# Fused attention and two expert layers on one core: zero rows and negated maxima in one transfer, x placed in two halves, early weights in every second step

## What is computed

```python
q_assign = argmax(q_n @ c_n.T); k_assign = argmax(k_n @ c_n.T)      # 16 clusters per head
scores = where(q_assign[:, None] == k_assign[None, :], q @ k.T / 8, -1e9)
attn = exp(scores - max(scores)); attn = attn / (sum(attn) + 1e-9)
x = heads_side_by_side(attn @ v)                                    # [1536, 512]
h = x @ w_in; P = a0 + a1*h + a2*h^2 + a3*h^3; Q = 1 + |b0||h| + |b1|h^2
y = (P / (Q + 1e-6)) @ w_out                                        # w_in [512, 2048]
out = ((y @ w1) * (y @ w2)) @ w3 @ w4                               # w1, w2 [512, 1024]
```

## Time and profile before

| | |
|---|---|
| median of three runs | 756.98 us (756.45 to 760.11) |
| the profiled execution | 757.19 us, of which the trace spans 755.4 us |
| TensorE matmul busy | 724.8 us, 96% of the span |
| TensorE weight load busy | 593.2 us, 79% |
| VectorE busy | 500.1 us, 66% |
| ScalarE busy | 423.1 us, 56% |
| GpSimd busy | 363.0 us, 48% |
| mean granted TensorE clock | 0.995 of full |

### The profile page before, as it was taken

One profiled execution on the slowest core, in us unless ns is written; L12 is line 12 of the kernel. 1 busy time (PEld: TensorE's weight loads), 2 busy tenths in 40 slices (PEclk: granted clock), 3 DMA queues, 4 the chain that ended last, 5 costly groups with the idle time before them and its releaser, 6 DMA issues.

```text
span 755.4 us, 12741 instructions
## 1 busy us (share of the span) xinstructions
PE 724.8 (96%) x4849; PEld 593.2 (79%) x4849; DVE 500.1 (66%) x796; ACT 423.1 (56%) x750; POOL 363.0 (48%) x271
## 2 busy tenths in 40 slices
PE   4899999999999999999999999999999999999998
PEld 2567667667677788888888888878779999998886
DVE  6888778778874577677767686775875555544211
ACT  4366666666665788878666686773433333223221
POOL 4068678768776646652222223441636466551000
PEclk9899999999999999999999999999999999999999
DMA  7334645444331442000000021103100100000111
GB/s 156 66 92 124 161 127 142 123 103 124 97 83 40 140 133 77 1 1 1 0 1 1 1 98 70 57 1 112 56 29 19 38 29 29 29 1 15 56 43 56
DMA packets 67132, 47.75 MB, mean 63 GB/s; under 512 B 30880, under 2 KB 59392, under 8 KB 67072
## 3 DMA queue, kind: packets, MB, share of 16 engines
q1 hardware_dynamic: 67072, 46.94, 22.5%
HBM read 28.35 MB, written 3.15 MB: 42 GB/s over the span
## 4 chain that ended last, share of the span: by engine, by line
PE 79%; SPq 12%; DVE 3%; DMA 2%; issue 2%; ACT 2%; POOL 0%; DVEq 0%; ACTq 0%
PE psum L1129 77%; SPq L1069 5%; SPq L1051 2%; SPq L1028 1%; DMA OPS<-NMT 1%; SPq L1042 1%; DMA OPS<-OPS 1%; SPq L1035 1%; DVE psum L1645 1%; SPq L1043 1%; PE psum L1134 1%; SPq L1053 1%; ACT P L1425 1%; DMA RAWQK<-in_k 1%; PE psum L663 1%
## 5 line engine op out<-in xcount | busy, mean ns | idle before, releaser
L1129 PE MATMUL psum<-OPS 128*128 128x384 f32 x576 | 129.9, 362 | 15.3 <-DMA OPS<-NMT 9.2
L1129 PEld LDWEIGHTS psum<-OPS 128*128 128x128 f32 x576 | 98.6, 194 | 48.1 <-issue 19.3
L541 POOL TENSOR_TENSOR G<-TT,G 128x512 fp32r<-128x512 f32 x48 | 62.3, 1299 | 151.6 <-ACT G L426 151.6
L1807 POOL TENSOR_TENSOR PSUMS<-PSUMS,P 128x768 f32<-128x768 f32 x64 | 108.2, 1690 | 17.1 <-ACT P L1425 8.7
L1425 ACT ACTIVATE P<-psum 128x768 f32<-128x768 f32 x96 | 76.4, 810 | 55.6 <-PE psum L1129 55.3
L1645 DVE TENSOR_REDUCE psum<-psum 128x1 f32<-128x768 f32 x90 | 86.5, 961 | 28.7 <-PE psum L1129 28.1
L1129 PE MATMUL psum<-G,WSPLIT 128*128 128x512 f32 x360 | 86.6, 390 | 1.1 <-POOL G L541 1.1
L1129 PE MATMUL psum<-XT,WSPLIT 128*128 128x512 f32 x360 | 86.5, 389 | 0.0
L471 DVE SCALAR_TENSOR_TENSOR HH<-UU,ABSB,psum 128x512 f32<-128x512 f32 x48 | 35.9, 748 | 69.0 <-ACT TT L404 68.9
L1129 PEld LDWEIGHTS psum<-G,WSPLIT 128*128 128x128 f32 x360 | 67.4, 188 | 15.5 <-POOL G L541 1.5
L1129 PEld LDWEIGHTS psum<-XT,WSPLIT 128*128 128x128 f32 x360 | 67.6, 188 | 14.0
(11 more groups left out here) (126 smaller groups left out, 1257.9 us busy)
## 6 DMA issues: line engine op xcount, KB each, us to landing
OPS<-OPS SPq DMA_DIRECT2D x32, 192.0 KB, 3.3
W3R<-in_moe_w SPq DMA_DIRECT2D x8, 512.0 KB, 3.8
RAWF<-in_moe_w SPq DMA_DIRECT2D x16, 256.0 KB, 3.3
RAWQK<-in_q SPq DMA_DIRECT2D x16, 192.0 KB, 3.2
RAWQK<-in_k SPq DMA_DIRECT2D x16, 192.0 KB, 3.9
V<-in_v SPq DMA_DIRECT2D x16, 192.0 KB, 2.9
XT<-XH SPq DMA_DIRECT2D x64, 48.0 KB, 2.0
XT<-XL SPq DMA_DIRECT2D x64, 48.0 KB, 2.0
```

The lines of the kernel that those rows point to most:

```text
L541: nc.gpsimd.tensor_tensor(G[:, n % 2, 1, :], TT[:, n % 4, :], G[:, n % 2, 0, :].bitcast(F32), ALU.subtract).then_inc(g_lo, 1)
L1129: return nc.tensor.matmul(o, stationary, moving, start=start, stop=stop, skip_group_check=True)
L1807: nc.gpsimd.tensor_tensor(total, P32[:, (2 * u) % 4, :, 0:QS] if n == 1 else total, P32[:, (2 * u + n) % 4, :, 0:QS], ALU.add).then_inc(p_ ...
```

## The change

`place_masks` loses its DMA of zeros. In its stead BQ is taken out of OPS into a tile of its own, BQS, in which the slots of units u and u + 2 (two slots of the same parity) lie side by side. NM becomes four groups of six columns; `negate_maxima(u)` writes one of the two halves of a pair, and the other half stays zero from a memset at the start. The transpose, the copy and the DMA of `place_maxima` carry both halves: twelve rows of 128 in place of six, so that one DMA writes the negated maxima of unit u and zeros for unit u + 2.

In SyncE's step `copy_rows` comes first, then the XH half of `place_x`, `load_v`, `place_maxima`, the XL half of `place_x`, `load_qk`, weights, masks. The early weights 1 to 5 are loaded in steps 1, 3, 5, 7, 9 (before: 1 to 5). As BQ has moved, the waits of the later weights change: tile 8 waits for the scores of unit 14, tile 9 for those of unit 15, and tile 9 is issued behind `place_x(14)`.

```diff
-            AQ, AK, BQ, BK = range(4)
+            AQ, AK, BK, BQ = range(4)
-            OPS = ph("OPS", [P, 4, 4, S], F32R)
+            OPS = ph("OPS", [P, 4, 3, S], F32R)
+            BQS = ph("BQS", [P, 2, 2, S], F32R)
-            NM = ph("NM", [P, 8], F32)
+            NM = ph("NM", [P, 2, 2, NT], F32)
...
+        def operand(slot, which):
+
+            return BQS[:, slot % 2, slot // 2, :] if which == BQ else OPS[:, slot, which, :]
...
-            return TP[0:NT, 0, 0:P] if 2 <= u <= UNITS - 2 else SM[0:NT, 0, 0:P]
+            return TP[0:2 * NT, 0, 0:P] if 2 <= u <= UNITS - 2 else SM[0:2 * NT, 0, 0:P]
...
+            if f == 8:
+                sp.wait_ge(st_ready, NT * (UNITS - 1))
             if f == 9:
-                sp.wait_ge(st_ready, NT * (UNITS - 1))
-            if f == 10:
                 sp.wait_ge(st_ready, NT * UNITS)
...
-                sp.dma_start(OPS[96:97, u % 4, BQ, :].bitcast(F32), OPS[97:98, u % 4, BQ, :].bitcast(F32)).then_inc(mask_rows, 16)
...
-                sp.dma_start(OPS[96:97, u % 4, BQ, :].rearrange("j (n w) -> j n w", n=NT).bitcast(F32),
-                             NMT[0:NT, :].bitcast(F32)).then_inc(nm_rows, 16)
-
-            def place_x(u):
+                sp.dma_start(BQS[96:97, u % 2].rearrange("j s (n w) -> j (s n) w", n=NT).bitcast(F32),
+                             NMT[0:2 * NT, :].bitcast(F32)).then_inc(nm_rows, 16)
+
+            def place_x(u, parts=((0, XH), (1, XL))):
...
             def step(u):
-                if has(u - 2):
-                    place_x(u - 2)
                 if has(u + 3):
                     copy_rows(u + 3)
+                if has(u - 2):
+                    place_x(u - 2, ((0, XH),))
                 load_v(u + 1)
                 place_maxima(u + 1)
+                if has(u - 2):
+                    place_x(u - 2, ((1, XL),))
                 if has(u + 5):
                     load_qk(u + 5)
-                if u < EARLY_W:
-                    load_weights(sp, u, ld_w[u])
+                if u % 2 == 1 and u < 2 * EARLY_W - 2:
+                    load_weights(sp, (u + 1) // 2, ld_w[(u + 1) // 2])
                 if has(u + 3):
                     place_masks(u + 3)
...
-            load_later_weights(sp, 9)
             place_x(UNITS - 2)
-            for f in range(10, 14):
+            for f in range(9, 14):
                 load_later_weights(sp, f)
...
-                        pe.wait_ge(mask_rows, 80 * (u - DIRECT + 1))
+                        pe.wait_ge(mask_rows, 64 * (u - DIRECT + 1))
...
-                nc.tensor.transpose(turn_bank(u), NM[:, 0:NT], IDENT).then_inc(nm_turned, 1)
+                nc.tensor.transpose(turn_bank(u), NM[:, u // 2 % 2].rearrange("p s n -> p (s n)"), IDENT).then_inc(nm_turned, 1)
...
-                nc.scalar.copy(NMT[0:NT, :], turn_bank(u)).then_inc(nm_copied, 1)
+                nc.scalar.copy(NMT[0:2 * NT, :], turn_bank(u)).then_inc(nm_copied, 1)
...
+            nc.vector.memset(NM, 0.0).then_inc(nm_cleared, 1)
...
-                nc.vector.tensor_scalar(NM[:, 0:NT], rows, -1.0, CAP, ALU.mult, ALU.min).then_inc(nm_ready, 1)
+                nc.vector.tensor_scalar(NM[:, u // 2 % 2, u // 2 % 2], rows, -1.0, CAP, ALU.mult, ALU.min).then_inc(nm_ready, 1)
...
-                nc.gpsimd.memset(OPS[96:P, slot, BQ:BK + 1, :].bitcast(F32), 0.0).then_inc(ops_const, 1)
+                nc.gpsimd.memset(operand(slot, BQ)[96:P].bitcast(F32), 0.0)
+                nc.gpsimd.memset(operand(slot, BK)[96:P].bitcast(F32), 0.0).then_inc(ops_const, 1)
```

More of the change, by code:

```diff
@@ L98, in build @@
             VMEAN = ph("VMEAN", [P, 2], F32)
-            NM = ph("NM", [P, 8], F32)
-            ph("GAP_P", [P, 39 + 207], F32)
+            NM = ph("NM", [P, 2, 2, NT], F32)
+            ph("GAP_P", [P, 39 + 207 - 16], F32)
             ph("GAP_HH", [P, 5 * CH], F32)
@@ L197, in build @@
         nm_ready = sem("nm_ready")
+        nm_cleared = sem("nm_cleared")
         nm_turned = sem("nm_turned")
@@ L1041, in copy_rows @@
                 slot = u % 4
-                sp.dma_start(OPS[0:D, slot, BQ, :].bitcast(F32), OPS[0:D, slot, AQ, :].bitcast(F32)).then_inc(b_rows[slot], 16)
+                sp.dma_start(operand(slot, BQ)[0:D].bitcast(F32), OPS[0:D, slot, AQ, :].bitcast(F32)).then_inc(b_rows[slot], 16)
                 sp.dma_start(OPS[0:D, slot, BK, :].bitcast(F32), OPS[D:P, slot, AK, :].bitcast(F32)).then_inc(b_rows[slot], 16)
@@ L1050, in place_masks @@
                         part = (2 * side + x) * QUAD
-                        sp.dma_start(OPS[D:D + QUAD, u % 4, which, x * HALF:(x + 1) * HALF].bitcast(F32),
+                        sp.dma_start(operand(u % 4, which)[D:D + QUAD, x * HALF:(x + 1) * HALF].bitcast(F32),
                                      MROWS[part:part + QUAD, :].bitcast(F32)).then_inc(mask_rows, 16)
-                sp.dma_start(OPS[96:97, u % 4, BQ, :].bitcast(F32), OPS[97:98, u % 4, BQ, :].bitcast(F32)).then_inc(mask_rows, 16)
             def place_maxima(u):
@@ L1059, in place_maxima @@
                     sp.wait_ge(ops_const, 2 * 4)
-                sp.dma_start(OPS[96:97, u % 4, BQ, :].rearrange("j (n w) -> j n w", n=NT).bitcast(F32),
-                             NMT[0:NT, :].bitcast(F32)).then_inc(nm_rows, 16)
-            def place_x(u):
+                sp.dma_start(BQS[96:97, u % 2].rearrange("j s (n w) -> j (s n) w", n=NT).bitcast(F32),
+                             NMT[0:2 * NT, :].bitcast(F32)).then_inc(nm_rows, 16)
+            def place_x(u, parts=((0, XH), (1, XL))):
                 sp.wait_ge(x_done, u + 1)
                 to = slice(u % 2 * D, u % 2 * D + D)
-                for e, src in ((0, XH), (1, XL)):
+                for e, src in parts:
                     for g in range(4):
@@ L1137, in ops @@
             def ops(u, which):
-                return OPS[:, u % 4, which, :]
+                return operand(u % 4, which)
             def sides(u):
@@ L1383, in ops2 @@
             def ops2(u, which, rows=slice(0, P)):
-                return OPS[rows, u % 4, which, :].rearrange("p (h n) -> p h n", h=2)
+                return operand(u % 4, which)[rows].rearrange("p (h n) -> p h n", h=2)
             def round_q(u):
@@ L1404, in scale_masks @@
                     if u > DIRECT:
-                        act.wait_ge(mask_rows, 80 * (u - DIRECT))
+                        act.wait_ge(mask_rows, 64 * (u - DIRECT))
                     last = nc.scalar.activation(MROWS, SIM, ACT.Copy, scale=BIG_ROOT)
@@ L1648, in negate_maxima @@
                 rows = MROW0 if u == 0 else MROW
+                if u == 0:
+                    dve.wait_ge(nm_cleared, 1)
                 dve.wait_ge(sm_free, NT * (u + 1))
```

## The result

The changed kernel takes 747.82 us (median, 747.38 to 748.13), the kernel before in the same runs 756.72. The ratio is 0.9877, interval 0.9849 to 0.9904. Forecast was 748.0. The profiled execution took 748.09 us (forecast for it: 748.3) with a span of 746.3. One of the six executions of the later run `e9_cen_later` took 4041.28 us, for which there is no trace; its ratio leaves it out.

The account below looks back on a forecast made before the run. SyncE's DMA queue, slower per attention step than TensorE's 13.5 us, was taken as the bound. 757.19 - 9.2 of waits + 0.3 gave 748.3 profiled, 748.0 against the median, range 746.8 to 751.8.

Parts of the forecast that it names:

- What bounds: Attention: SyncE's queue step, 14.82 us with weights and 13.59 without, exceeds TensorE's 13.5, so the maxima's DMA is late.
- Zero row, order and weights: SyncE's step: 0.64 us less per step, maxima 2.64 us earlier, weights spread to 27.13 us a pair against 26.96.
- Maxima before XL: SyncE's step: the maxima's DMA is issued 1.1 us early at worst, so all eight waits go, 9.2 us.
- The transfer of twelve rows: DMA of the negated maxima: taken as 2.40 us, between 2.1 and 2.9, with 0.83 us of issue.
- The masks: Needed by `score_max(u + 3, 0)` at 11.80 us, landing at 10.07, or 11.14 with the stall; 0.7 to 1.7 left.
- rival 3: Attention: masks become the bound and the kernel slower, 764.5 us if they land 1.5 us late; chance 0.04.
- Rival 2: TensorE's wait for the maxima is the transfer's own 2.40 us, so all eight waits stay, 756.5 to 757; chance 0.06.
- the rule of the cheap dispatch: SyncE's queue: issuing is cheap, some 50 ns, so taking 13 issues away gives under 1 us and the maxima stay late.
- Costs taken as nothing: Transpose 0 to 1.3 us, copy at most 0.26 again, memsets and later weights: each taken as 0.

Follow-up runs that it names:

- e9_cen_later: The changed kernel with q and k of unit 0 loaded ahead of the centroids; 748.1 us, ratio 0.9866.
- e7: The changed kernel with one more DMA of 3 KB behind the maxima in steps 1 to 12; 751.03 us, ratio 0.9918.
- e8: The changed kernel with two more DMAs of 3 KB a step behind the maxima in steps 1 to 12; 756.66 us, ratio 0.9996.
- e3: The kernel before with only the zero row merged into the transfer of the maxima, old order and weights' steps; 753.2 us, ratio 0.9948.
- e4: The changed kernel with the early weights back in steps 1 to 5; 749.17 us, ratio 0.989.
- e5: The changed kernel with SyncE's step in the old order, both halves of x ahead of the maxima; 753.84 us, ratio 0.9953.
- e6: The changed kernel with both halves of x behind the maxima; 762.14 us, ratio 1.0056.
- e2: The kernel before with only the early weights moved to steps 1, 3, 5, 7, 9; 757.88 us, ratio 1.0002.
- e10: The changed kernel as it is, run again; 747.41 us, ratio 0.9859.
- e1: The kernel before with only the new order of SyncE's step; 751.33 us, ratio 0.9912.

## Why the prediction was right, point by point

*What bounds: the queue's step against TensorE's 13.5.* Right for the steps with weights, where the queue had no pause of over 0.2 us from 78 to 134 us and four waits made 5.3 of the 9.2 us. Misread for the steps without: the prediction took 13.59 against 13.5 as a lateness that stays, but ahead of the three waits there, and of that at 74.46, the queue had stood idle for MROWS, and these 3.8 us come from the place of the maxima behind the masks and x. The change removes both, since it shortens the list by 0.64 us and this path by 0.64 + 2.64; that both came out of one forecast is in part luck. Adding 0.6 us a step costs 3.2 us in all, 1.2 us a step brings back the old time (e7, e8, by way of the masks); taking 0.64 away alone gives 3.9 us (e3, 757.12 to 753.2).

*Zero row, order and weights.* The sum was right, and the parts were not priced one by one. By their effect alone they are 3.9 (zero row), 5.8 (order: 757.12 to 751.33) and nothing that can be told; the first two together 7.9 (e4) and not 9.7, as they act on the same eight waits.

*Maxima before XL, 1.1 us of margin in the heaviest case.* The queue's part was right: the DMA was issued 96.23 - 82.46 = 13.77 us after the last copy's end, forecast 14.18 at worst, and in all steps from 55 us on it left within 0.63 us of its own copy's end. That x must be split is shown by e5 (waits for the maxima) and e6 (waits at `score_max(u + 2, 0)`).

*The transfer of twelve rows, taken at 2.40, bounded by 2.9.* Mis-sized in its upper end. Where TensorE was stopped by it, the time from issue to restart can be read. In the traces of e3, e5, e7 and the changed kernel there are fifteen such cases: nine lie from 2.30 to 2.54, six at 3.05, 3.33, and 3.86 to 4.10. With six rows, in sixteen cases of the kernel before and of e2, it was 2.04 to 2.43. In e10 there is one more, of 3.59. (Only transfers that stopped TensorE can be read so, and those of the changed kernel stop it only when they take over 4 us, so these counts don't tell how often a landing is late.) At 4.10 the margin is gone, which is the one wait of 0.2 in the changed kernel: issued at 123.06, TensorE went on at

```profile
127.16 0.62 PE L1135 MATMUL psum<-BQS,OPS 128*128 128x384 f32 x2 [0.21 <-DMA BQS<-NMT]
```

The forecast came out since the DMA is issued early enough in all steps; it stood nearer to the edge than the text said. Four of the late ones (3.86, 3.90, 3.94, 4.10) are the same transfer, issued between 123 and 126.1 us, in four kernels, which speaks for something else that runs there; twice the rows as the cause was not tested either. So this stays open. The issue itself cost 0.82 for 0.78, as taken.

*The masks, landing at 10.07 to 11.14 against 11.80.* The mechanism was right, the landing too short: I took the median of 2.1. In the changed kernel the last one is issued at 90.4, 7.9 after the copy (forecast 7.97), and the masks of that step take 2.7 to 3.2 to land, so that the last is there between 10.6 and 11.1, with 0.7 to 1.2 of margin and not 1.7. Steps without weights have up to 3.1, so the 512 KB of weights ahead are not shown to be the reason. In the step of 163.31 the margin was gone: with stalls in XL and k the last mask was issued 9.2 after the copy's end, and TensorE started `score_max` at 175.35, 12.04 after it and not 11.80. That is the wait of 0.3. The bound of 11.14 was therefore too low, and the change runs at this edge as well. e6, 2.6 us later, is over it: rival 3 is a real mechanism. That my price for it (1.5 us in each of eleven steps, 764.5) was near what e6 showed (762.14) is luck, for e6 has five waits of 0.2 to 3.3 us and a slower clock behind some of them.

*Rival 2 and the rule of the cheap dispatch.* Rival 2 is refuted by the result and by e1: the waits for NMT went while the transfer got no shorter. The rule is refuted by e7 and e8: a DMA holds this queue for about 0.6 us whatever its size (0.58 for 3 KB, 0.60 for 192 KB), and that of twelve rows onto one partition for 0.82. By the Trainium skill's "usually small relative to the DMA itself" ("DMA: Bandwidth & Descriptors", section "Issuing engines are not separate DMA queues") the added DMAs would change little; the traces disagree, with 0.58 us of issue beside median landings of 2.0 (e7) and 1.7 (e8) for these DMAs, and the time rose by 3.2 and 8.8 us. The 50 ns that the prediction takes from that page of the Trainium skill stand there for DMAs issued from GpSimd, and these are issued from SyncE.

*Costs taken as nothing.* The transpose with twelve columns took 85 ns of weight load for 83, the copy 257 for 255, and the later weights brought no wait after attention.

## What to carry to other kernels

Add up the issues of a DMA queue over one turn of the loop and compare the sum with the turn of the busiest engine: here 21 issues, most of 0.6 us, and one stall of some 1.1 were 14.8 against 13.5, and no row of busy time shows it. Look too at where the list waits: a wait in its middle (here for the masks' rows) delays what stands behind it even when the list is short enough. Shorten the list first, then place in it, right behind the wait, the transfer that is needed next, and leave on each side only as much as its own deadline allows; both deadlines have to be worked out, for the wait moves to the other one (e5, e6). A margin should be reckoned with the landing times and the stalls of its own stretch, and not with the median over the whole trace.

## What the runs showed of the hardware that I had not expected

After the wait of 3.32 us in e6 TensorE's granted clock was at 0.50 (1.2 GHz) from 100 to 102 us, and after that of 2.76 in e1 it was 0.64 on average from 112 to 115; after the waits of 1.90 us in the kernel before and 1.83 in e6 (at 158.32) it stayed at 1.00 (2.4 GHz). The length of the wait alone doesn't decide it: after 2.36 us in e7 (at 178.15) and 2.58 in e8 (at 155.79) it stayed at 1.00 as well, while after 2.23 in e6 (at 127.99) it was at 0.50 from 130 to 132. What decides it was not found. In e6 the step after the wait of 3.32 took 113.72 - 98.67 = 15.05 us from copy to copy against 13.43, with no wait of its own in the timeline, so a wait of 3.3 cost nearly 5. This goes with e6 and e8 losing more than their waits (16.2 for 10.6, and 11.4 for 8.9 us).

A transfer of 3 KB behind 512 KB of weights and four mask DMAs of 48 KB took 4.4 us to land (e1), against a median of 1.8 in the kernel before. So a small transfer can land as late as a large one; whether it would have landed sooner ahead of the large ones was not tested.
